# A routed expert layer on one core: half-slot code in six sizes, gates out of a one-hot matmul, and matmuls on constants while rows are gathered

## The reference, cut to what matters

```python
# attention: q, k, v are (4, 8, 576, 64); 4 heads with a plain window of 32, 4 with a dilated one
x = attention(q, k, v)                      # -> (2304, 512)
# experts: D = 512, E = 8, F = 1024
logits = x @ w_gate
e_idx = argmax(logits, axis=1)              # one expert for each token
gate_w = softmax(logits)[n, e_idx]          # divisor: sum of exponentials + 1e-9
eom = sigmoid(x @ w_output_gate)
for e in range(8):
    mask = e_idx == e
    h = maximum(x[mask] @ w1[e], 0)
    out[mask] = gate_w[mask, None] * eom[mask, e, None] * (h @ w2[e])
# MLP: 512 -> 2048 -> 512
h = out @ w_in
g = maximum(h, 0) + log1p(exp(-abs(h)))
y = g @ w_out
```

## Time and profile before

| | us |
|---|---|
| median of three runs | 832.69 |
| lowest, highest | 825.91, 837.83 |
| the profiled execution's own time | 831.72 |
| its span | 829.9 |
| PE busy | 770.0 (93%) |
| DVE, ACT, POOL busy | 424.5, 410.0, 173.3 |

### The profile page before, as it was taken

The page is one execution under the profiler, slowest core; times in us unless marked ns, Lnnn a source line. Parts: engine busy times, 40 slices in busy tenths (PEclk is TensorE's granted clock), DMA queues, the critical chain, the costliest instruction groups (busy, mean ns, idle before and its releaser), DMA issues.

```text
span 829.9 us, 13450 instructions
## 1 busy us (share of the span) xinstructions
PE 770.0 (93%) x4640; PEld 695.9 (84%) x4641; DVE 424.5 (51%) x854; ACT 410.0 (49%) x1041; POOL 173.3 (21%) x172
## 2 busy tenths in 40 slices
PE   5999995498989999999679999999999999999996
PEld 3667664498989999999669999999989999999995
DVE  8885986754534667665345343334343334334332
ACT  3885984244544566745345353344335335335332
POOL 6220220543360547634100010010001001001001
PEclk9999997599999999999879999999999999999999
DMA  9567502235443566755300010000000000000000
GB/s 261 160 187 270 203 0 114 77 131 174 142 166 132 196 220 200 230 176 199 130 2 1 0 39 0 0 25 13 0 0 38 0 0 38 0 0 38 0 0 38
DMA packets 27890, 74.70 MB, mean 90 GB/s; under 512 B 4737, under 2 KB 12945, under 8 KB 27345
## 3 DMA queue, kind: packets, MB, share of 16 engines
q1 hardware_dynamic: 20624, 53.52, 19.6%
q0 software_dynamic: 6224, 16.03, 5.9%
q10 hardware_dynamic: 1008, 4.73, 1.4%
HBM read 64.81 MB, written 9.46 MB: 89 GB/s over the span
## 4 chain that ended last, share of the span: by engine, by line
PE 89%; DVE 6%; issue 3%; ACT 1%; POOL 0%; ACTq 0%; DVEq 0%
PE bank L564 13%; PE bank L566 13%; PE bank L565 13%; PE bank L587 8%; PE bank L589 8%; PE bank L585 8%; PE bank L574 4%; PE bank L578 4%; PE bank L576 4%; PE bank L452 4%; PE bank L476 2%; PE bank L489 2%; PE bank L462 2%; PE bank L553 1%; PE bank L448 1%
## 5 line engine op out<-in xcount | busy, mean ns | idle before, releaser
L1099 DVE SCALAR_TENSOR_TENSOR g_sb<-bank,soft 128x384 f32<-128x384 f32 x96 | 53.5, 557 | 239.8 <-ACT soft L839 239.8
L835 ACT ACTIVATE soft<-bank 128x384 f32<-128x384 f32 x96 | 47.3, 492 | 213.9 <-PE bank L566 213.9
L564 PE MATMUL bank<-x_hi,w_hi 128*128 128x384 f32 (+2 forms) x448 | 145.6, 325 | 7.1 <-issue 6.0
L566 PE MATMUL bank<-x_hi,w_lo 128*128 128x384 f32 (+2 forms) x448 | 144.8, 323 | 0.0
L565 PE MATMUL bank<-x_lo,w_hi 128*128 128x384 f32 (+2 forms) x448 | 144.6, 323 | 0.0
L1053 DVE TENSOR_TENSOR w_lo<-raw,w_hi 128x1024 fp32r<-128x1024 f32 x72 | 98.0, 1365 | 31.3 <-ACT w_hi L761 30.3
L424 POOL DMA_INDIRECT out<-y_sb,out_rows_i x18 | 17.3, 963 | 413.8 <-ACT y_sb L846 410.2
L564 PEld LDWEIGHTS bank<-x_hi,w_hi 128*128 128x128 f32 x448 | 85.4, 191 | 10.7 <-issue 6.8
L565 PEld LDWEIGHTS bank<-x_lo,w_hi 128*128 128x128 f32 x448 | 85.4, 191 | 2.1
L566 PEld LDWEIGHTS bank<-x_hi,w_lo 128*128 128x128 f32 x448 | 85.2, 190 | 0.0
L790 ACT ACTIVATE h_hi<-bank 128x384 fp32r<-128x384 f32 x64 | 31.5, 492 | 101.1 <-PE bank L566 101.0
(11 more groups left out here) (165 smaller groups left out, 1569.1 us busy)
## 6 DMA issues: line engine op xcount, KB each, us to landing
raw<-we SPq DMA_DIRECT2D x64, 512.0 KB, 3.5
x_tokens<-x_sb ACTq DMA_DIRECT2D x6, 768.0 KB, 5.1
v_sb<-vw SPq DMA_DIRECT2D x4, 1024.0 KB, 11.8
raw_m<-wm POOLq DMA_DIRECT2D x8, 512.0 KB, 4.1
raw<-wm SPq DMA_DIRECT2D x8, 512.0 KB, 3.5
q_sb<-qT SPq DMA_DIRECT2D x4, 768.0 KB, 8.4
k_sb<-kT SPq DMA_DIRECT2D x8, 384.0 KB, 10.1
v_sb<-vw SPq DMA_DIRECT2D x4, 512.0 KB, 4.6
```

Of the source, the lines that this page charges most:

```text
L564: nc.tensor.matmul(bank_[:, 0:rows], hi[:, w], x_hi[:, k, 0:rows], start=(k == 0), stop=False)
L566: last = nc.tensor.matmul(bank_[:, 0:rows], lo[:, w], x_hi[:, k, 0:rows], start=False, stop=(k == KC - 1))
```

## The change

- The code of a slot is written for half a slot (four chunks), in six sizes (384, 352, 320, 288, 256, 224), and stands in a loop of two halves inside one loop over all 13 slots with an If for the unused ones. The extra copy for overflow slots is gone.
- The weight ring has four chunks; high, low and raw parts have buffers of their own, and splits run three chunks ahead. SP waits for the low split and not for the products. `yT_ps` is cleared by DVE before each slot (`zero_y`), since a half's first product no longer starts a sum.
- The next slot's rows come as two halves of 256 columns, are scaled by POOL (`scale_half`), and are transposed in the middle of each half slot. There are two sets of x parts, chosen by the slot's parity, an index known at run time.
- The gates no longer go through DRAM. DVE cuts them into three BF16 pieces, multiplies them with the block matrix and PE sums them by `place_onehot` (18 matmuls), as it does with the sources. The sources use two BF16 digits in place of one F16 number.
- DVE's order behind the sources is another: half indices, pieces of the gates, the slots' experts, summed gates, scaling of the first rows and clearing, sizes, three weight splits with the first rows' low parts, and only then starts, positions and the loads of registers.
- PE runs matmuls on constants into a spare part of bank 0: 24 when the gates are there, and 16 after each of the first two blocks of transposes.
- Further: `expert_order` is scattered after all slots, and 8 MLP chunks come through the ring behind the last slot; four of them get their high parts in buffers of the finished slots.

```diff
-SIZES = (SLOT, 320, 256)
+SIZES = (SLOT, 352, 320, 288, 256, 224)
-RING = FC1
-AHEAD = 4
-HRING = 4
-KEPT = FC2 - RING
+RING = 4
+HALF = FC1 // RING
+AHEAD = RING - 1
+HRING = 3
+KEPT = FC1
+TAIL = FC2 - KEPT
...
@@ POOL
+            def scale_half(slot, h):
+                q = 2 * (slot - 1) + h
+                pool.wait_ge(halves_loaded[h], 16 * TPS * slot)
+                if q:
+                    pool.wait_ge(rows_t_done, FIRST_T + 2 * q)
...
+                    nc.gpsimd.tensor_scalar(xs_sb[:, j, :], landing[:, j, h, :], row_scale[:, c:c + 1], None, ALU.mult
+                                            ).then_inc(rows_scaled, 1)
...
+            for s in range(1, E + 1):
+                for h in range(2):
+                    scale_half(s, h)
+                    if s < E:
+                        halves_scaled(s, h)
+                        load_half(s + 1, h)
+                    elif not h:
+                        split_mlp_chunk(s - 2)
+                    if s == 1 and not h:
+                        pool.wait_ge(sizes_ready, 1)
+                        used = overflow_slots(pool)
+                        pool.wait_ge(positions_ready, 1)
+                    if not h:
+                        load_mlp_chunk(s - 1)
+                    elif 1 < s < E:
+                        split_mlp_chunk(s - 2)
...
@@ PE
+            pe.wait_ge(block_scales, 1)
+            for t in range(NT):
+                last = nc.tensor.matmul(scale_ps[:, 0:PIECES * BLOCKS], place_onehot[:, :, t], block_scale[:, :, :, t],
+                                        start=(t == 0), stop=(t == NT - 1))
+            last.then_inc(scales_summed, 1)
+            def keep_running(n):
+                for _ in range(n):
+                    nc.tensor.matmul(bank[0][:, SLOT:SLOT + P], ones_b[:, :], lower_b[:, :], start=True, stop=True,
+                                     skip_group_check=True)
             def first_transposes():
+                pe.wait_ge(row_scales_ready, 1)
+                keep_running(24)
                 for j in range(TPS):
-                    pe.wait_ge(rows_scaled, j + 1)
+                    pe.wait_ge(first_scaled, j + 1)
...
+                    if j < TPS - 1:
+                        keep_running(16)
+            def half_slot_products(slot, half, parity, rows):
+                first = slot * FC1 + half * RING
...
+                p1(0)
+                p1(1)
+                p2(0)
+                p1(2)
+                pe.wait_ge(x_lo_done, slot * KC + half * 2 + FIRST_X)
+                pe.wait_ge(rows_scaled, slot * (2 * TPS) + half * TPS + TPS)
+                transpose_rows(0)
+                p2(1)
+                p1(3)
+                transpose_rows(1)
+                p2(2)
+                p2(3)
+            def slot_products(slot):
                 taken = pe.value_load(taken_i[0:1, bass.ds(slot, 1)], min_val=0, max_val=N)
+                parity = slot % 2
+                def from_size(half, n):
...
+                with pe.Fori(0, HALF) as half:
+                    from_size(half, 0)
+            first_transposes()
+            pe.wait_ge(sizes_ready, 2)
+            used = overflow_slots(pe)
+            with pe.Fori(0, SLOTS) as slot:
+                with pe.If(slot < used + E):
+                    slot_products(slot)
...
@@ DVE
+            step(V.tensor_copy(source_part[:, :], source_ps[:, BLOCKS:IDS * BLOCKS]))
+            step(V.scalar_tensor_tensor(source[:, :], source_ps[:, 0:BLOCKS], float(NT), source_part[:, :],
+                                        ALU.mult, ALU.add))
             V.tensor_copy(source_i[:, :], source[:, :]).then_inc(sources_ready, 1)
...
+            split_lo(0, 1)
+            for k in range(KC):
+                row_lo(slice(0, 1), k, first_t_ps[k], k + 1)
+            split_lo(1, 2)
+            split_lo(2, 3)
...
+            def slot_parts(slot):
+                other = bass.ds((slot + 1) % 2, 1)
+                for f in range(FC1):
+                    dve.wait_ge(h_hi_done, slot * FC1 + (f + 1))
...
+                    if f % RING >= 2:
+                        k = f // RING * 2 + f % RING - 2
+                        row_lo(other, k, t_ps[k % 2], slot * KC + (FIRST_X + k + 1))
+                    c = f + AHEAD
+                    split_lo(c % RING, slot * FC1 + (c + 1))
+                for k in range(KC):
+                    dve.wait_ge(y_copied, slot * KC + (k + 1 + PLACE_CREDIT))
+                    zero_y(k)
...
@@ ACT
+                    act.wait_ge(g2_done, slot * FC1 + (c - RING + 1 + G2_CREDIT))
+                    split_hi(c % RING, raw_loaded[c % RING], slot * (16 * HALF) + 16 * (c // RING + 1), w_hi_done)
```

More of the change, by code:

```diff
@@ L134, in build @@
         route = {n: sb(early, f"route_{n}", [P, NT]) for n in
-                 ("m", "first", "sum", "z", "ez", "den", "dest", "shift", "position", "index")}
+                 ("m", "first", "sum", "z", "ez", "den", "scale", "rest", "dest", "shift", "position", "index")}
         routee = {n: sb(early, f"routee_{n}", [P, NT, E]) for n in
@@ L557, in product1, with transpose_rows, x_part @@
-            def product1(bank_, hi, lo, done, rows=SLOT, x_done=None):
+                    if j < TPS - 1:
+                        keep_running(16)
+            def transpose_rows(n):
+                for j in range(TPS):
+                    last = nc.tensor.transpose(t_ps[n][:, P * j:P * (j + 1)], xs_sb[:, j, P * n:P * (n + 1)],
+                                               ident[:, :])
+                last.then_inc(rows_t_done, 1)
+            def product1(bank_, hi, lo, done, rows, parity, x_done=None):
+                def x_part(n, k):
+                    return x_parts[:, parity, n:n + 1, k:k + 1, 0:rows].rearrange("p a n k r -> p (a n k r)")
@@ L622, in _, with p1, p2 @@
-            first_transposes()
-            pe.wait_ge(route_done, 1)
-            used = overflow_slots(pe)
-            def sized_slot(slot):
+            def half_slot_products(slot, half, parity, rows):
+                first = slot * FC1 + half * RING
+                def p1(i):
+                    pe.wait_ge(w_lo_done, first + (i + 1))
+                    pe.wait_ge(h_lo_done, first + (i - 2 + 1 + H_CREDIT))
+                    product1(h_ps[i % 2], w_hi[:, i, :], w_lo[:, i, :], g1_done, rows, bass.ds(parity, 1),
+                             (x_lo_done, slot * KC) if i == 0 else None)
+                def p2(i):
+                    pe.wait_ge(h_lo_done, first + (i + 1 + H_CREDIT))
+                    product2_columns(i, w_hi[:, i, :], w_lo[:, i, :], g2_done, rows, slot * KC if i == 0 else None)
+                p1(0)
[10 more added lines that the diff above has]
+                p2(3)
@@ L776, in _, with row_part @@
-            for j in range(TPS):
-                act.wait_ge(first_rows[j], 32)
-                scale_rows(0, j)
-            def rows_hi(first, ks, banks):
-                for k in ks:
-                    act.wait_ge(rows_t_done, first + (k + 1))
-                    nc.scalar.activation(x_hi[:, k, :], banks[k % len(banks)][:, 0:SLOT], ACT.Copy).then_inc(x_hi_done, 1)
-            def slot_parts(slot, ahead):
-                start = act.value_load(start_i[0:1, bass.ds(slot, 1)], min_val=0, max_val=N)
+            def row_part(parity, n, k):
+                return x_parts[:, parity, n:n + 1, k, :].rearrange("p a n r -> p (a n r)")
@@ L1009, in _ @@
             V.tensor_copy(source_i[:, :], source[:, :]).then_inc(sources_ready, 1)
+            step(V.tensor_scalar(half_source_i[:, 0, :], source[:, :], 2.0, None, ALU.mult))
+            V.tensor_scalar(half_source_i[:, 1, :], source[:, :], 2.0, 1.0, ALU.mult, ALU.add
+                            ).then_inc(half_sources_ready, 1)
+            step(V.tensor_copy(scale_piece[:, 0, :], R["scale"][:, :]))
+            step(V.tensor_tensor(R["rest"][:, :], R["scale"][:, :], scale_piece[:, 0, :], ALU.subtract))
```

397 lines of the change are left out of this document (201 added, 196 removed).

## The result

| | before | after |
|---|---|---|
| median, us | 831.75 (4 runs) | 856.71 (4 runs, 855.62 to 858.43) |
| the profiled execution's span | 829.9 | 853.8 |
| PE starts the slots' products | 160.7 | 165.5 |
| last product of the slots | 407.3 | 437.6 |
| first product of the MLP | 420.4 | 443.0 |

The changed kernel is slower: ratio 1.030, 95% interval 1.022 to 1.038. The forecast was 839 in a range of 822 to 858, so the time lies near the range's upper end, and outside "within 2%", to which the forecast gave 0.72; slower had 0.22. The span grew by 23.9 us: 4.8 before the first product, 25.7 in the slots, 7.8 less behind them, and 1.3 in the MLP.

The account below looks back on a forecast made before the run. TensorE, busy 93% of the span, was taken as the bound, so only its own instructions or pauses count. The terms -9 + 6 + 9 + 6 - 8 + 3 = +7 on 831.72 us gave 839, range 822 to 858.

Parts of the forecast that it names:

- within 2%: Whole kernel: a time that can't be told from no change, 816 to 849.3 us; chance 0.72.
- sizes: PE's slot products: 280 and 278 tokens go from 320 to 288 columns, 196 and 203 from 256 to 224; -9 us.
- start: Before the first second-layer product: DVE's new order delays it from 166.7 to 171.2, plus slow clock; +6 us.
- first jumps: PE's first far jumps into half-slot bodies: slow ones and lost clock cost 13.5 us against 7.3 today; +6 us.
- chains of branches: Between halves and slots: branches over other sizes' bodies outlast the sequencer's lead, mostly around 224 columns; +9 us.
- leaving the slots: From last slot to MLP: the loop ends in code already passed, so PE starts at 412.0, not 420.44; -8 us.
- the rest: In the slots: register steps for the parity +2, Pool engine's scaling and DVE's added work +1; together +3 us.
- rival 4: Slot products: smaller sizes don't shorten them since loading weights sets the pace; -5 instead of -9, 843 us; forecast included, 0.55.
- rival 2: Half-slot bodies no longer stay loaded, each half pays at least one slow jump; 885 us, with two 944; chance 0.08.
- Rival 3: Small slots: DVE becomes the bound with Pool operations in its way, PE gaps grow 3 to 4 us; 853 us; chance 0.13.
- Rival 1: Slots: code is fetched ahead and branch chains are covered; 827 us, 808 with every end good; chance 0.24.

Follow-up runs that it names:

- a: The changed kernel without its 56 matmuls on constants; 871.81 us, ratio 1.032 to the original kernel.
- b: The changed kernel with DVE's 15 steps for starts and positions moved behind the second chunk of slot 0; 867.89 us, ratio 1.027 to the original kernel.
- g: The original kernel with four whole-slot sizes (384, 320, 288, 224) in one loop of 13 slots with an If; 888.99 us, ratio 1.069.
- h: The original kernel with four whole-slot sizes in one loop of 13 slots, smallest size asked first; 877.01 us, ratio 1.056.
- e: The changed kernel with its chain of Ifs turned round, smallest size asked first; 845.46 us, ratio 1.013 to the original kernel.
- c: The changed kernel with four sizes (384, 320, 288, 224) instead of six; 853.19 us, ratio 1.011 to the original kernel.
- d: The original kernel with its overflow slots run in one loop of 13 slots with an If; 840.68 us beside 844.56, ratio 0.996.
- f: The changed kernel with a single size, 384, for all half slots and no Ifs choosing sizes; 865.93 us, ratio 1.042 to the original kernel.
- l: The changed kernel, unchanged, repeated as a control on a second chip; 854.42 us, ratio 1.026 to the original kernel.

## Why the prediction was right or wrong, step by step

| step | predicted | found |
|---|---|---|
| sizes | -9 | -8.8 |
| start | +6 | +9.3 |
| first jumps | +6 | +10.6 |
| chains of branches | +9 | +17.5 |
| leaving the slots | -8 | -7.8 |
| the rest | +3 | some +3 |
| sum | +7 | +24 |

The span grew by 23.9. The right column comes from the trace of after: pauses less the ordinary distance, and the clock's loss put to the pause ahead of it.

By kind instead of by place, most of the miss is clock and chain: half clock costs 10.1 us where 2.65 were counted (1.3 and 1.35), and the pauses of the chains and h_lo in the steady part cost 16.2 where 9.3 were counted.

**Sizes: right, and rival 4 was half true.** 320 to 288 gave 384 x (0.1466 - 0.1317) = 5.7 us. 256 to 224 gave 384 x (0.120 - 0.112) = 3.1 where 0.0133 a product would give 5.1: below 256 the distance shrinks by 0.008 and not by 0.0133. Whether the loading of weights sets this floor, as rival 4 has it, no run shows.

**Start: mechanism right, too small.** The 9.3 are 6.6 of delay and 2.7 of clock. The first second-layer product stood at 173.3 behind h_lo, predicted 171.2, because the first product itself stood at 165.5 and not at 161.9. More than half of that is the 18 gate matmuls: they were priced at 2.2 us and took 4.35 (151.66 to 156.01), at half clock:

```profile
151.70:156.00 4.30, 4.30 (x18) 2.46 (x18) 0.88 (x4) 0.00 (x0) 3.39 (x4) 0.50 0.67 186
```

The 2.7 us of slow clock behind it were put at 1.3. That the constants gain nothing held (a). That the pause matters didn't quite: b removed it and the time stayed, with a longer pause at the first jump (4.06 for 2.70) and one more stretch of half clock.

**First jumps: the right kind, the clock under-sized.** Slow jumps were forecast between the halves of slot 0, from slot 0 to 1 and into the 320 body; they came between the halves of slot 0, from slot 0 to 1 and between the halves of slot 1 (228.55), and none at 320: three slow branches, where the 7.3 us from slot 0 to 1 had counted two and the whole four. The pauses less the ordinary distance sum to 11.9 us, near the forecast without the clock (12.2). That agreement is in part luck, since 7.3 at one place became 3.9 and a pause of 5.5 stood where none was forecast. The clock was counted once (1.35) and fell after all three: 1.6 + 2.5 + 2.0 = 6.1 us. The fetches stopped at 234.7, and rival 2, code that no longer stays loaded, didn't happen: the interval 240 to 440 has none. Whether it does is a matter of size, as g and h show: fetches in nearly every slot, pauses up to 18 us, and 5.6 to 6.9% of the time, of the order of its 6% (839 + 46).

The Trainium skill, "Runtime: NRT & Kernel Launch", section "Instruction fetch mechanics", says two things of the size: that PE has 128 KiB, 2048 instructions, and, of the memory in general, that it is two lines of 16 KiB and that a taken branch out of a window of two pages forces a fetch. The prediction used only the second, and its remark that the trace doesn't agree concerns that one. The runs agree with the first as far as 1410: loops of 1290 and 1410 instructions, jumped over in each slot, fetch nothing on q8 from 240 on. They fall short of it in g, where 1720, still under 2048, are fetched again; at which count it turns, and why below 2048, no run here shows.

**Chains of branches: the term that was mis-sized most,** 9 against 17.5. e and c show that these pauses follow the chain: they vanish or shrink with the levels before them, with the same products. Where a pause was forecast it came. Four were 0.3 to 0.7 us longer: 2.2 from 320 to 224 (1.5), 1.6 between the halves of 224 (1.3), 3.0 from 224 to 224 (2.6) and 2.3 from 224 to 288 (1.9). The fifth was 1.95 from 288 to 320 (0.7). Five pauses stood where none was forecast: 0.8 from 288 to 384, 0.5 from 384 to 320 and 0.65 between the halves of 288, which had been taken as covered, and two waits of 0.8 for h_lo in the 224 slots; and one more stretch of slow clock, 1.3. The two waits for h_lo stay in e (0.8 each, 1.6 together), so they are DVE's and not the chain's; without them and the clock the chains are 14.6.

The trace splits the miss between the chain and its cover. At the end of a half the sequencer takes the loop's step (L694). In the first 224 slot it does so here:

```profile
L694 PEldq ALU_OP  x1: 32/32/32, 329.7 to 329.7; - x1
```

The half's last product starts at 330.97 and the next half's first at 332.73, so the sequencer was 1.24 us ahead, as forecast (1.3), but the chain took 3.0 us and not 2.6. Between slots it took 4.3 and not 3.9. The price of a level was right (0.4, shown by c); the fixed part, with its register steps, was 0.4 to 0.6 short behind the bodies of 224. At the larger sizes the cover was short as well: 1.2 to 1.6 us at 288 (forecast 2.3), 2.0 at 320 (2.7) and 2.65 at 384 (3). It had been worked out from how far the sequencer was ahead in 384 and 256 bodies of whole slots.

**Leaving the slots: right in size and in what came next.** The pause is 5.65 us instead of 13.46, ended by the low part of the MLP's rows. d does it to the kernel before alone: 5.2. Part of what is left is DVE's own five empty turns over unused slots, which the chain shows from 439.7 to 442.4, between its last clearing and that low part.

**The rest: right in size.** f bounds it at 384 columns: no pause from the ring, the Pool engine or the parity. The longer first one of three second-layer products gives some 2 us by the durations above, an estimate, and the MLP has 1.3 more. Rival 3 (DVE becomes the bound in small slots, +14) didn't happen: DVE's mean split rose from 1.37 to 1.40 us, and the waits for h_lo in the 224 slots are 0.8 us twice.

Rival 1, fetched ahead and covered, is refuted by the same rows. The forecast's sign of every term was right. It counted the clock behind two pauses where there were five, and gave the chains 0 to +16, where the truth lay just above. That the total still fell into the stated range is owed to the range's width, 36 us: three of the six terms came out high and none low enough to make up for them.

## What to carry to other kernels

More sizes of unrolled code are bought with branches: count how many bodies the sequencer must step over between two pieces of work, and whether the work behind it lasts as long as that chain; ask first for the size whose work is shortest, and write no size that the data don't use (c: 12 to 16 us for two entries of a list; other inputs may need them). Then count the instructions of the whole loop: here 1410 stayed loaded, and 1720 made the kernel 57 us slower. And a pause on TensorE costs its length and, often, half clock behind it: the five pauses above 2.6 us in the slots of after had it behind them, while in l one of 4.0 us had none and two of 2.1 and 2.4 had it. A fix that removes one pause has to be measured at the next.

## What the runs showed of the hardware that was not expected

On the chip of a to d, ScalarE started late after TensorE had ended. In c, with the last product at 420.8, its two waits near the end of slot 7 were

```profile
ACT yT_sb L850 <- remote: 11.2, 1, 11.2
ACT w_hi L820 <- remote: 6.6, 1, 6.6
```

where "remote" says that the profile found no instruction that released it; in the seven slots before, the copy of yT followed the products within a microsecond. a and b show the same at that place, d shows five pauses of 0.8 to 2.6 us inside slots instead, in the unchanged order of the kernel before. The Pool engine was issuing indirect transfers each time, 18 in a row in c, but after and l have the same burst at the same place without the delay. So it depends on the chip or on the moment; the cause stays open. The kernel before is 12 us slower on that chip too (844.56 against 832), and the ratios of a and b are those of after; whether the same delay is behind both isn't shown.

A fetch of code costs more than its transfer. The seven of 16 KB between 160 and 240 in after took 0.6% of 16 engines' 80 us, 1.1 us each. The three slow branches, each with one such fetch inside it (188.1, 211.4, 231.2), took 3.0 to 5.0; over all kernels slow branches took 1.4 to 7.8 us.

The constants brought PE's clock to 1.00 for the first products, and the pause of 3.75 us behind them took it back to 0.50: work without use buys the clock only up to the next pause. In b, which hasn't that pause, it held to 188.9; in l it fell at 168.3, behind 2.4 us in which PE waited for the first rows.
